# A mask on ScalarE, masks and odd queries on other queues, a first step put off, and TensorE waits moved ahead, in a fused attention and two-MLP kernel

## The reference

```
for t in range(S):                                   # B, H, S, D = 4, 8, 768, 48
    cur = einsum('bhd,bhe->bhde', u * k[t], v[t])
    y[:, :, t] = einsum('bhd,bhde->bhe', r[t], state + cur)
    state = w[t][..., None] * state + einsum('bhd,bhe->bhde', k[t], v[t])
x = y.transpose(0, 2, 1, 3).reshape(3072, 384)
x = (x @ w_a) * (x @ w_b) @ w_out                    # 384 -> 1536 -> 384
h = x @ w_in2
out = (max(h, 0) + alpha * min(h, 0)) @ w_out2       # 384 -> 2048 -> 384
```

## Time and profile before

| what | value |
|---|---|
| median of 3 runs | 1011.1 us (1010.41 to 1011.45) |
| profiled execution, its own time | 1010.97 us |
| its span | 1009.2 us |
| TensorE matmuls busy | 987.4 us, 98% |
| VectorE busy | 586.3 us, 58% |
| ScalarE busy | 296.8 us, 29% |
| GpSimd busy | 24.1 us, 2% |
| mean granted TensorE clock | 0.998 |

### The profile page before, as it was taken

The page is one execution under the profiler, slowest core; times in us unless marked ns, Lnnn a source line. Parts: engine busy times, 40 slices in busy tenths (PEclk is TensorE's granted clock), DMA queues, the critical chain, the costliest instruction groups (busy, mean ns, idle before and its releaser), DMA issues.

```text
span 1009.2 us, 26702 instructions
## 1 busy us (share of the span) xinstructions
PE 987.4 (98%) x11200; PEld 963.8 (96%) x11200; DVE 586.3 (58%) x1209; ACT 296.8 (29%) x628; POOL 24.1 (2%) x24
## 2 busy tenths in 40 slices
PE   5799999999999999999999999999999999999998
PEld 5799999999999999999999999999999999999998
DVE  7796765855857658567432437555555555555554
ACT  3435314223242242341223324222222222222212
POOL 4400000000000000000000000000000000000000
PEclk9999999999999999999999999999999999999999
DMA  6554311312113013110020414010101010101000
GB/s 174 144 149 121 93 38 34 111 30 65 53 29 92 25 36 87 53 37 2 25 60 15 128 32 126 8 40 11 38 13 35 13 34 14 32 16 32 20 6 23
DMA packets 42126, 52.88 MB, mean 52 GB/s; under 512 B 5152, under 2 KB 42016, under 8 KB 42016
## 3 DMA queue, kind: packets, MB, share of 16 engines
q1 hardware_dynamic: 40624, 51.04, 17.7%
q10 hardware_dynamic: 1392, 0.25, 0.2%
HBM read 39.48 MB, written 9.44 MB: 48 GB/s over the span
## 4 chain that ended last, share of the span: by engine, by line
PE 95%; DVE 3%; issue 1%; ACT 0%; ACTq 0%; DMA 0%; DVEq 0%; SPq 0%
PE products L170 18%; PE products L172 16%; PE products L171 16%; PE acc L170 12%; PE acc L171 12%; PE acc L172 12%; PE products L740 3%; PE products L758 1%; PE products L800 1%; PE products L816 1%; PE products L715 1%; PE products L785 1%; PE products L772 1%; DVE f_y L986 1%; DVE k_in L998 1%
## 5 line engine op out<-in xcount | busy, mean ns | idle before, releaser
L170 PE MATMUL products<-x_parts,weights_hi 128*128 128x384 f32 x576 | 202.2, 351 | 2.6 <-DMA x_parts<-f_y 2.0
L172 PE MATMUL products<-x_parts,weights_lo 128*128 128x384 f32 x576 | 195.1, 339 | 0.3 <-issue 0.3
L171 PE MATMUL products<-x_parts,weights_hi 128*128 128x384 f32 x576 | 194.7, 338 | 0.0
L1375 DVE TENSOR_SCALAR leaky_low<-products,leaky_al 128x384 f32<-128x384 f32 x128 | 79.1, 618 | 169.9 <-PE products L172 169.8
L1322 ACT ACTIVATE leaky_g_hi<-leaky_g_sb 128x384 fp32r<-128x384 f32 x128 | 67.3, 526 | 295.5 <-DVE leaky_g_sb L1380 183.8
L1235 DVE TENSOR_TENSOR g_sb<-a_g,products 128x384 f32<-128x384 f32 x96 | 53.1, 553 | 158.9 <-issue 90.8
L549 ACT ACTIVATE g_hi<-g_sb 128x384 fp32r<-128x384 f32 x96 | 50.3, 524 | 254.5 <-DVE g_sb L1235 254.5
L170 PEld LDWEIGHTS products<-x_parts,weights_hi 128*128 128x128 f32 x576 | 108.0, 187 | 7.8 <-issue 2.7
L172 PEld LDWEIGHTS products<-x_parts,weights_lo 128*128 128x128 f32 x576 | 108.2, 188 | 0.7 <-issue 0.7
L171 PEld LDWEIGHTS products<-x_parts,weights_hi 128*128 128x128 f32 x576 | 108.2, 188 | 0.0
L170 PE MATMUL acc<-g_hi,weights_hi 128*128 128x384 f32 x288 | 96.6, 336 | 0.0
(11 more groups left out here) (94 smaller groups left out, 1757.4 us busy)
## 6 DMA issues: line engine op xcount, KB each, us to landing
k_in<-in_k_dram SPq DMA_DIRECT2D x16, 336.0 KB, 3.9
r_in<-in_r_dram SPq DMA_DIRECT2D x16, 336.0 KB, 5.2
stage<-in_w_out_dram SPq DMA_DIRECT2D x14, 384.0 KB, 3.3
w_v<-in_v_dram SPq DMA_DIRECT2D x16, 288.0 KB, 3.6
y_dram<-x_in SPq DMA_DIRECT2D x8, 576.0 KB, 4.6
x_in<-y_dram SPq DMA_DIRECT2D x8, 576.0 KB, 4.6
out_dram<-leaky_out_sb SPq DMA_DIRECT2D x7, 576.0 KB, 3.3
stage<-in_w_dram SPq DMA_DIRECT2D x10, 336.0 KB, 3.8
```

What stands on the lines that cost most here:

```text
L170: pe.matmul(out, w_hi, x_hi, start=first, stop=False)
L171: pe.matmul(out, w_hi, x_lo, start=False, stop=False)
L172: return pe.matmul(out, w_lo, x_hi, start=False, stop=last)
L1375: dve.tensor_scalar(self.low[f % 2][:, :], h, 0.0, self.al[:, f:f + 1], ALU.min, ALU.mult).then_inc(self.low_ready, 1)
```

## The change

1. ScalarE copies `four_mask` (`copy_four_mask`) behind its preparation of round 0, where VectorE copied it in phase 7 of round 0.
2. The two loads of `level_mask` are issued by SyncE behind its six loads of keys, queries and decays; ScalarE issued them before.
3. In round 0, stream 0, VectorE copies the odd queries to `r_leaf`, which ScalarE did. TensorE's leaf and GpSimd's first step wait for it (`odd_copied`).
4. In round 0 VectorE makes the products of decays of levels 2 and 3 for each stream by itself (`APART`, with other counts in `f_count`).
5. In round 2 the first steps of stream 1 come later: `step_r` behind `prepare_fours(2, 0)`, `first_step_k` behind `merge_fours(2, 0)`.
6. The low part of piece 6 (`PUT_OFF`) is taken in slot 2 between `g_sb` and `g_lo`, where it was taken at the end of slot 1.
7. The five waits of `four` are a function, `wait_four`, called in `up_b(g)` ahead of its last block of products, in every round from 2 on and for both streams.

```diff
@@ def f_count(duo, index, j):
-    if duo == 0:
-        return j + 1 if index == 0 else index + 2
+    if duo == 0 and index < APART:
+        return APART * j + index + 1
     if duo < FOURS_FROM:
-        return 6 * duo + index + 2
-    return 12 * duo - 6 * FOURS_FROM + (7 if j == 0 else 1) + index + 1
+        return 6 * duo + index + APART + 1
+    return 12 * duo - 6 * FOURS_FROM + (8 if j == 0 else 2) + index + APART - 1
@@ SyncE
                 load_w(0, 1)
+                for hd in range(2):
+                    rows = slice(64 * hd, 64 * hd + 64)
+                    sp.dma_start(view(level_mask, 0, [[32, len(MASKED)], [1, 32]], 64, 64 * hd),
+                                  constants[rows, 3 * P:(3 + len(MASKED)) * P].rearrange("p (m q) -> p m q", q=P)[:, :, 32 * hd:32 * hd + 32]).then_inc(masks_loaded, 16)
                 sp.wait_ge(w_loaded[1], 16)
@@ GpSimd, step_r
                         pool.wait_ge(r_prepared[j], n + 1)
+                        if j == 0:
+                            pool.wait_ge(odd_copied, 1)
@@ ScalarE, prepare_r
-                    copy(every_other(r_leaf[j], 1), every_other(queries_of(n, j), 1))
+                    if n > 0 or j > 0:
+                        copy(every_other(r_leaf[j], 1), every_other(queries_of(n, j), 1))
@@ ScalarE
-                for hd in range(2):
-                    rows = slice(64 * hd, 64 * hd + 64)
-                    act.dma_start(view(level_mask, 0, [[32, len(MASKED)], [1, 32]], 64, 64 * hd),
...
                 act.dma_start(ident[:, :], constants[0:ROWS, 0:ROWS]).then_inc(ident_loaded, 16)
+                copy_four_mask()
@@ TensorE, leaf
+                    if n == 0 and j == 0:
+                        pe.wait_ge(odd_copied, 1)
@@ TensorE
-                def four(n, j, g):
+                def wait_four(n, j):
 
                     pe.wait_ge(merged, merges(n, 0, 3))
                     pe.wait_ge(fours_merged, fours(n, j))
                     pe.wait_ge(k_first[j], n + 1)
                     pe.wait_ge(fours_copied[j], fours_round(n))
                     pe.wait_ge(fours_stepped[j], 2 * fours_round(n))
+
+                def four(n, j, g):
+
@@ TensorE, up_b
                             for block in range(KT):
                                 wait_x(tile + 1, block)
+                        if kt == KT - 1 and step_at(g) is not None:
+                            n, phase = divmod(step_at(g), PHASES)
+                            if n >= FOURS_FROM and phase in (2, 3):
+                                wait_four(n, phase - 2)
                         product = up_part(g, "w_b", b_ps(g), kt)
@@ VectorE, attend
                         if n == 2:
-                            first_steps(n)
+                            first_steps(n, 0)
...
                         if n >= FOURS_FROM:
                             prepare_fours(n, 0)
+                        if n == 2:
+                            step_r(n, 1, 0)
                     elif phase == 2 and n >= FOURS_FROM:
                         merge_fours(n, 0)
+                        if n == 2:
+                            first_step_k(n, 1)
                         prepare_fours(n, 1)
...
-                    elif phase == 7 and n == 0:
-                        copy_four_mask()
@@ VectorE, round 0
+                dve.wait_ge(r_loaded[0], 16)
+                dve.tensor_copy(every_other(r_leaf[0], 1), every_other(queries_of(0, 0), 1)).then_inc(odd_copied, 1)
                 first_step_k(0, 0)
...
                 merge_leaf(0, 0)
+                products_of_w(0, 0, 1, (2, 3))
                 step_k(0, 0, 1)
                 first_step_k(0, 1)
-                products_of_w(0, 1, 1, (1,))
-                products_of_w(0, 0, 2, (2,))
+                products_of_w(0, 1, 1, (1, 2))
...
-                products_of_w(0, 0, 2, range(3, 7))
+                products_of_w(0, 1, 1, (3,))
+                products_of_w(0, 0, 2, range(4, 7))
@@ VectorE, slots
                         attend_early(step)
+                    if g == 2:
+                        shared.split_lo(dve, PUT_OFF)
...
                         for piece in new_pieces(f):
-                            shared.split_lo(dve, piece)
+                            if piece != PUT_OFF:
+                                shared.split_lo(dve, piece)
```

More of the change, by code:

```diff
@@ L43 @@
 FIRST_NEW = [5, 5, 7, 9, 10, 11, 13, 15, 16, 17, 18, 18, 18]
+PUT_OFF = 6
 STAGED_FROM = 3
+APART = 3
 FOUR = 2
@@ L327, in halves, with every_other @@
                 return view(tile, side * h, [[2 * h, S // (2 * h)], [1, h]])
+            def every_other(tile, side):
+                return view(tile, side, [[2, S // 2]])
             def decays_of(n):
@@ L556, in scaled @@
                     return done
-                def every_other(tile, side):
-                    return view(tile, side, [[2, S // 2]])
                 def prepare_k(n, j):
@@ L573, in prepare_r, with copy_four_mask @@
                         act.wait_ge(products_done[j], after(n - 1, 2))
-                    copy(every_other(r_leaf[j], 1), every_other(queries_of(n, j), 1))
+                    if n > 0 or j > 0:
+                        copy(every_other(r_leaf[j], 1), every_other(queries_of(n, j), 1))
                     scaled(r_leaf[j], queries_of(n, j), 0, j).then_inc(r_prepared[j], 1)
+                def copy_four_mask():
+                    act.wait_ge(masks_loaded, 32)
+                    dims = [2 * FOUR, Q // (2 * FOUR)]
+                    copy(view(four_mask, 0, [dims, [FOUR, 2], [1, FOUR]], P),
+                         view(level_mask, 0, [dims, [0, 2], [1, FOUR]], P)).then_inc(four_mask_ready, 1)
                 def copy_fours(n, j):
@@ L655, in _ @@
                     act.dma_start(leaf_mask[rows, :], constants[rows, P + 64 * hd:P + 64 * hd + BLOCK]).then_inc(leaf_mask_loaded, 16)
-                for hd in range(2):
-                    rows = slice(64 * hd, 64 * hd + 64)
-                    act.dma_start(view(level_mask, 0, [[32, len(MASKED)], [1, 32]], 64, 64 * hd),
-                                  constants[rows, 3 * P:(3 + len(MASKED)) * P].rearrange("p (m q) -> p m q", q=P)[:, :, 32 * hd:32 * hd + 32]).then_inc(masks_loaded, 16)
                 act.wait_ge(warmed, 1)
@@ L1127, in step_r, with first_steps @@
                     dve.tensor_tensor(halves(t, h, 1), halves(t, h, 1), decay(n, j, h, 0), ALU.mult).then_inc(r_stepped[j], 1)
-                def first_steps(n):
-                    for j in range(2):
-                        first_step_k(n, j)
-                        step_r(n, j, 0)
+                def first_steps(n, j):
+                    first_step_k(n, j)
+                    step_r(n, j, 0)
                 def lower_outputs(n):
@@ L1163, in attend @@
                         if n == 1:
-                            first_steps(n)
+                            first_steps(n, 0)
+                            first_steps(n, 1)
                         products_of_w(n, 0, 2 if n < FOURS_FROM else 1, range(1, 7))
@@ L1190, in attend @@
                         copy_last_level(n)
-                    elif phase == 7 and n == 0:
-                        copy_four_mask()
-                    elif phase == 7:
+                    elif phase == 7 and n > 0:
                         step_r(n, 0, 5)
```

7 lines of the change are left out of this document (1 added, 6 removed).

## The result

| | before | after |
|---|---|---|
| median of 5 runs | 1011.1 us (1010.41 to 1012.33) | 1028.21 us (1026.83 to 1030.55) |
| profiled execution, its span | 1010.97 us, 1009.2 us | 1028.21 us, 1026.4 us |
| mean granted TensorE clock | 0.998 | 0.993 |

After to before is 1.0167, with an interval of 1.015 to 1.0184: slower by 17 us. All five runs have a mean clock of 0.992 or 0.993. The forecast was 1019.8 us and its range ended at 1024.0. The sign was right; 8.8 us were forecast and 17.2 came.

What follows compares the result with a forecast made beforehand. TensorE bounds the kernel, its matmuls covering 987.4 of 1009.2 us. Start -3.2, slot 2 -0.5, rounds 3 to 7 +11.0 and round 2 +1.5 give +8.8 us: 1019.8 us, range 1017.0 to 1024.0.

Steps and rivals of the forecast that it cites:

- The moved waits: Rounds 3 to 7: TensorE stands ahead of `up_b`'s last block until VectorE ends `prepare_fours`, 2.2 us each, +11.0 us.
- Stream 1 at nothing: Stream 1's wait moves one block; VectorE is done 0.9 us before TensorE comes to it, so no cost.
- Round 2: Earlier `g_sb` wins the 0.7 us wait at `four`, but the moved wait makes `four` 1.5 us later in all.
- the bound of 116.10: Round 2: the earliest time, in us, at which TensorE's own products allow `g_sb` to start, against 116.78 before.
- the rival: New pauses cost the clock: one to six falls to 1.2 GHz, 1.7 us each, 1021.5 to 1030 us; 13%.
- The start: Changes 1 to 4, up to the first tile's first product: 3.2 us earlier, ends 1.9 and 4.1.
- The chain of 1.2 us: Round 0's chain VectorE, GpSimd, TensorE gets 1.2 us shorter by earlier leaf and changed VectorE order; 0.4 to 1.7.
- The mask's 1.9 us: Without VectorE's copy of `four_mask` the states start at 30.8 and not 32.7, 1.9 us earlier.
- The clock behind the states: Round 0: a shorter wait for the states may leave TensorE at 2.4 GHz, or slow clock lasts longer; 0 to 1 us.
- The cap by SyncE's queue: SyncE's queue has 2.1 us to give before the moves; with the chain's 1.2 the start gains at most 3.3 us.
- Slot 2: Change 6 takes one low part from ahead of `g_sb`, removing TensorE's 0.5 us wait; ends 0 and 0.5.
- The rival that it is faster: Moved wait stops nothing, 1006.6 us, 10%; decided by whether `prepare_fours` ends by 186.0 in round 3.

Runs made afterwards that it cites:

- the two other places: Kernel before with stream 0 and 1's five waits between `up_b` and `down`: 1023.88 us; or ahead of `up_b`'s second block: 1034.14 us.

## Why the prediction failed, step by step

**The moved waits, 11.0 us (10.0 to 11.5): right.** Six pauses of 2.24 us, at the places and with the releaser named, five of which are 11.2 us. The reason given (VectorE's path doesn't hang on TensorE in that stretch) is borne out by the 4.49 us of round 3, and the two other places moved the pauses by a block as it says. Stream 1 at nothing: right, by the kernel that moved it alone.

**Round 2, 1.5 us (1.0 to 2.0): right but for the clock.** 3.10 us came, of which 1.7 are a fall of the clock. Change 5 won what was forecast: the bound of 116.10 is 116.72 with the lag of 0.62 us, and `g_sb` started at 116.69, released by TensorE's product.

**The clock: the failed step.** The forecast set the fall at nothing and gave the rival 13%. It had two rows: 3.2 us with a fall and 1.97 without, and it called 2.2 us nearer to the second. That is true of the distance and says nothing, since nothing lay between. The profiles of the kernels with moved waits showed that pauses in between go either way: with TensorE idle for 1.7 us it fell behind none of five pauses (though two of that kernel's four runs hold more falls than its profile); for 2.1 us behind five of eleven (three of six after, two of five with the waits alone); for 2.35 us and more behind six of eight. Three falls in the MLP are what the rival had priced (1.7 us each, 1024 for two or three, 1030 for six); a fourth stood in the start, where no rival had put one. The price was 1.5 to 1.7 us each. The 1028.2 us lie within the 1021.5 to 1030 of this rival, but in part by luck: its mechanism brought 4.7 of the 8.4 us that were missing, and most of the rest is the start.

**The start, -3.2 us (-1.9 to -4.1): failed, +0.48 came.** By the forecast's own terms its ends should have been 2.3 (0.4 of the chain and 1.9 of the mask) and its cap of 3.3. Term by term:

- The chain of 1.2 us: the sign was wrong, the keys were turned 0.63 us later. The decays landed 0.9 us later than in the profile before (first step on them at 7.61 and not 6.68), and from that step to the turn of the keys only 0.3 us were won (19.84 against 20.14). The two engines still held each other up: GpSimd's first step now starts with VectorE's, and VectorE's next product is stretched to 1.52 us, where it took 0.55 at 7.16 before. The forecast's sum had counted only the collision that goes.

```profile
8.08 1.52 DVE L1009 TENSOR_TENSOR f_y<-w_v 112x384 f32<-112x384 f32 x1
```

- The mask's 1.9 us: 1.71 came against this profile. Against an execution with the short copy it would have been nothing, so the term was luck of the profile.
- The clock behind the states, 0 to 1 us: 1.14 came.
- The cap by SyncE's queue: the right queue and the wrong size. The forecast said that its loads hang on GpSimd's low parts and let these move ahead with the chain; they came later, at 29.66 against 29.03, and the loads with them. SyncE came to the moves at 38.53, right behind the piece (38.42). From the end of the outputs to the first product it then took 1.17 us more than before.
- The fall behind the wait ahead of the first tile, at nothing in the forecast: 1.5 us.

The first product so came at 42.94, 2.1 us behind the 40.8. The chain is 1.8 of the missing 3.7 us, the way from the outputs to the first product 1.2, the fall 1.5 and the mask 0.2; the clock behind the states gave about 1.1 back.

**Slot 2, -0.5 us (-0.5 to 0): failed, +0.14 came.** The wait for `g_sb` went, as written. The step that failed is that the whole wait was counted as won: the next release, `a_g` in slot 3, had come 0.1 us ahead of TensorE before the change and stood still behind the rounding of piece 8. The later load that the forecast priced at nothing is that of another piece (9), and no wait of TensorE's names it.

In sum 8.4 us were missing between 1019.8 and 1028.2. The start made 3.7 of them, slot 2 0.6, and the rounds 4.1 (three falls of 4.7 us together, less the 0.5 us gap of before near 240).

**The rival that it is faster:** its point of decision was right. `prepare_fours` ended behind the new place, and TensorE stood.

## What to carry to other kernels

On an engine that works in order, a wait is moved ahead only as far as its releaser's end in the trace allows; from there on each product moved behind it is a product that no longer covers. Price such a pause with the clock as well: where the trace holds one pause that kept it and a longer one that lost it, anything between is open, and the range has to take in a fall for each. When a wait is taken away, look at how close the next release on the same engine was, since the gain ends there. And read the duration of an instruction that runs beside another engine's from several executions before it becomes a term, for the same copy lasted 1.04 or 4.61 us.

The version that beats both kernels is changes 1 to 6 with the waits at `four` and `a_g` ahead of piece 8: 1008.25 us, 0.9981 of before; the same kernel with one edit more or less gave 0.9972 to 0.9981 in three further comparisons.

## What was not expected of the hardware

- Pauses of equal length (2.24 us between products) in the same program were followed by 1.2 GHz at 121.5, 193.2 and 401.4 us and not at the other three. What makes the difference wasn't found.
- Ahead of the first tile, waits up to 1.97 us were never followed by a fall (7 profiles) and waits of 2.1 us and more always (6 profiles). Within the MLP the same lengths go either way.
- A VectorE copy beside a row of GpSimd instructions lasted 1.04 or 4.61 us by a start of 28.08 or 28.05 us, with GpSimd's times alike to 0.01 us (1.05 us with a start at 28.06 in the kernel with changes 5 and 6). In the kernel with the waits one block earlier it was 4.61 us again, with a start at 28.03.
- The kernel before ran from 1008.29 to 1013.62 us over 75 runs on three chips. The mean clock tells part of it: 30 runs at 1.000 have a median of 1010.9 us, 29 at 0.998 one of 1010.1 us, and 15 at 0.997 one of 1011.8 us. So one fall more or less doesn't set the time, two go with a longer one, and the rest of the spread has another cause, of which the copy may be one; that wasn't measured.
